# The buffer of x rounded up to a multiple of 2 KB per partition

## The reference

```python
# 1 attention with decay, in blocks of 64 tokens
intra = (q_b @ k_b.T * Dmask) @ v_b
inter = (q_b * lam_pow) @ kv_state
out_b = intra + inter
kv_state = lam_block * kv_state + (k_b * rev_pow).T @ v_b

# 2 gated feed-forward with token shift (d_model 512, d_ff 1024)
xk = mu_k * x + (1 - mu_k) * x_prev          # x_prev: x one token earlier
xr = mu_r * x + (1 - mu_r) * x_prev
x = sigmoid(xr @ w_r) * (max(xk @ w_k, 0) ** 2 @ w_v)

# 3 gate from a causal convolution of 5 taps
gate = sigmoid(sum(conv_w[j] * x shifted by 4 - j tokens))
out = (gate * (x @ w_val)) @ w_out
```

## Time and profile before

| | |
|---|---|
| time, median of 3 runs | 307.41 us (306.47 to 308.93) |
| the profiled execution | 305.9 us |
| its span, first to last instruction | 304.0 us |
| TensorE matmul in flight | 286.8 us, 94% |
| VectorE busy | 164.6 us, 54% |
| ScalarE busy | 118.8 us, 39% |
| GpSimd busy | 48.1 us, 16% |
| granted TensorE clock, mean | 0.983 |

### The profile page before, as it was taken

How to read it: one execution, slowest core, us unless ns; L and a number is a source line. 1 busy time by engine, 2 the same in 40 slices (tenths; PEclk the granted TensorE clock), 3 DMA queues, 4 the chain that set the end, 5 groups by cost and what they waited for, 6 DMA issues and landing times.

```text
span 304.0 us, 4295 instructions
## 1 busy us (share of the span) xinstructions
PE 286.8 (94%) x1772; PEld 232.6 (77%) x1772; DVE 164.6 (54%) x251; ACT 118.8 (39%) x197; POOL 48.1 (16%) x38
## 2 busy tenths in 40 slices
PE   8998698999699999996999999789999999999996
PEld 8877586787488878875888888568887888887885
DVE  6547895298442004765444676621996879714100
ACT  1017624755362104645510155644711711612221
POOL 1684799950000000000000000000000000000000
PEclk9999899999799999999999999979999999999999
DMA  7999993000000000000000000070000000110122
GB/s 274 378 412 409 410 375 110 2 0 3 0 0 0 2 0 0 0 2 0 0 0 2 0 1 0 15 263 2 0 0 2 0 0 0 71 69 0 69 106 104
DMA packets 7506, 23.42 MB, mean 77 GB/s; under 512 B 832, under 2 KB 1216, under 8 KB 7488
## 3 DMA queue, kind: packets, MB, share of 16 engines
q1 hardware_dynamic: 7488, 23.16, 20.1%
HBM read 20.01 MB, written 3.15 MB: 76 GB/s over the span
## 4 chain that ended last, share of the span: by engine, by line
PE 90%; DVE 4%; DMA 3%; ACT 2%; issue 1%
PE ps L638 27%; PE ps L640 26%; PE ps L639 26%; PE ps L654 3%; PE ps L703 3%; DMA qk<-in_qk 3%; PE ps L781 2%; PE ps L671 1%; PE ps L688 1%; DVE xk_f L484 1%; DVE kk_f L499 1%; DVE pT L460 1%; DVE xr_l L490 1%; ACT ring L326 1%; DVE kk_l L504 1%
## 5 line engine op out<-in xcount | busy, mean ns | idle before, releaser
L638 PE MATMUL ps<-xk_h,wk_h 128*128 128x512 f32 x96 | 38.1, 397 | 0.8 <-issue 0.8
L639 PE MATMUL ps<-xk_l,wk_h 128*128 128x512 f32 x96 | 38.1, 396 | 0.0
L640 PE MATMUL ps<-kk_h,wv_l 128*128 128x512 f32 x96 | 38.1, 396 | 0.0
L638 PE MATMUL ps<-kk_h,wv_h 128*128 128x512 f32 x96 | 38.1, 396 | 0.0
L640 PE MATMUL ps<-xk_h,wk_l 128*128 128x512 f32 x96 | 38.0, 396 | 0.0
L639 PE MATMUL ps<-kk_l,wv_h 128*128 128x512 f32 x96 | 38.0, 396 | 0.0
L523 DVE SCALAR_TENSOR_TENSOR gate<-x,prm,gate 128x512 f32<-128x512 f32 x48 | 32.6, 746 | 0.0
L343 ACT ACTIVATE gate<-x,prm 128x512 f32<-128x512 f32 x12 | 8.7, 725 | 54.1 <-DVE x L509 54.1
L638 PE MATMUL ps<-xr_h,wr_h 128*128 128x512 f32 x48 | 20.7, 430 | 7.8 <-DVE xr_l L490 7.8
L499 DVE SCALAR_TENSOR_TENSOR kk_f<-ps,ring 128x512 f32<-128x512 f32 x24 | 16.5, 689 | 18.8 <-ACT ring L326 18.8
L509 DVE TENSOR_TENSOR x<-ps,r 128x512 f32<-128x512 f32 x12 | 8.3, 691 | 33.0 <-PE ps L640 33.0
(11 more groups left out here) (69 smaller groups left out, 525.1 us busy)
## 6 DMA issues: line engine op xcount, KB each, us to landing
qk<-in_qk SPq DMA_DIRECT2D x12, 512.0 KB, 7.0
kv<-in_kv SPq DMA_DIRECT2D x12, 512.0 KB, 7.9
out<-out_sb SPq DMA_DIRECT2D x11, 256.0 KB, 2.0
wk_raw<-in_w_k SPq DMA_DIRECT2D x4, 512.0 KB, 10.1
wv_raw<-in_w_v SPq DMA_DIRECT2D x4, 512.0 KB, 8.7
wr_raw<-in_w_r SPq DMA_DIRECT2D x2, 512.0 KB, 8.5
w_raw<-in_w_val SPq DMA_DIRECT2D x2, 512.0 KB, 4.5
w_raw<-in_w_out SPq DMA_DIRECT2D x2, 512.0 KB, 8.0
```

The source lines that it names most:

```text
L638: nc.tensor.matmul(to, left(0), right(0), start=(i == 0), stop=False)
L639: nc.tensor.matmul(to, left(0), right(1), start=False, stop=False)
L640: done = nc.tensor.matmul(to, left(1), right(0), start=False, stop=(i == last))
```

## The change

The size that x takes is rounded up to the next multiple of 2,048 bytes, from 24,736 to 26,624. All that is laid out behind x moves up by 1,888 bytes: xk, xr, kk, ring, r, own, prm and all that shares their places. The weights and x stay where they are. No instruction is added, taken away or moved.

```diff
@@ -64,7 +64,7 @@
         KB = 1024
         wk_at, wr_at, wv_at = take(32 * KB), take(16 * KB), take(32 * KB)
-        x_at = take(4 * KT * XW)
+        x_at = take(-(-4 * KT * XW // (2 * KB)) * 2 * KB)
         xk_at, xr_at, kk_at = take(16 * KB), take(16 * KB), take(32 * KB)
         ring_at, r_at = take(8 * KB), take(8 * KB)
         own_at = take(16 * KB)
```

## The result

| | before | changed |
|---|---|---|
| time, median | 306.94 us (4 runs, 304.76 to 308.93) | 298.72 us (4 runs, 297.34 to 300.98) |
| ratio | | 0.974, 95% interval 0.9691 to 0.9789 |
| profiled execution, its span | 305.9, 304.0 us | 297.34, 295.3 us |
| granted TensorE clock, mean | 0.983 | 0.988 |

The change makes the kernel 2.6% faster. I had forecast no change (307.4 us, with 305.1 to 309.2 as the range).

The account below looks back on a forecast made before the run. TensorE was taken as the bound: number of matmuls times start-to-start distance, plus seams. Every term was 0 us, so the forecast stayed at the earlier median, 307.4 us, range 305.1 to 309.2, with 0.84 for within 1%.

Parts of the forecast that it names:

- Four distances are sampled by the four values of n.: Hidden layer: 128-column blocks n were taken to sample four operand distances, with no interval differing by 10 ns in 2,810.
- the distance of its two operands: TensorE: changing the separation of moving and stationary operands within 2 KB was forecast at 0 us, bound +1.0.
- 864 matmuls x 0.9 = 0.8 us: TensorE: most that operand alignment could gain, from 233.3 ns in the projection against 234.2 in hidden; bound -0.8 us.
- The term of the absolute addresses: TensorE: moving operands going from 32 past a multiple of 64 bytes to a multiple was forecast at 0 us, bound -0.8.
- Half of those matmuls stand at distance 0 and pay nothing: Attention, `attend`: operands at distance 0 or 256 take 63.8 ns each, read as no price for distance 0.
- The line through the 256- and the 512-column pace: TensorE: 120 and 233.3 ns extrapolated to 63.3 ns for 128 columns, compared with 63.8 ns in `attend`.
- The rival with the right mechanism: All 996 full-width matmuls: the 21 ns excess is an address effect, removed by a common grid; 286.6 us, half 297; chance 0.05.
- The slower rival: TensorE: weight load and moving stream meet when operands are equal modulo 512 bytes; +3.8 us, 311.2 us; chance 0.05.
- The independence of the two reads: TensorE: weight load and moving stream have independent ports per the Trainium skill, making the price of their meeting 0.
- VectorE, ScalarE and GpSimd at 0: The three other compute engines: address changes forecast to cost 0 us, with a bound of -1.0 us for GpSimd.
- The DMA at 0: Loads of qk and kv: moved targets forecast at 0 us, bounds -0.7 and +0.7 us.
- The clock episodes: Receptance heads: lower granted clock loses 1.7 us each; two or more extra or fewer, chance 0.03 slower, 0.03 faster.

Follow-up runs that it names:

- the kernel with 64, 128, 256: Changed kernel with pads ahead of xk, xr and kk, giving operand distances 64 in hidden, 128 in receptance, 256 in value; 299.21 us.
- the kernel with 320, 384, 448: Changed kernel with pads ahead of xk, xr and kk, giving operand distances 320 in hidden, 384 in receptance, 448 in value; 305.01 us.

## Why the prediction was wrong

**"Four distances are sampled by the four values of n."** This is the step that failed. The blocks are 512 bytes apart, and the pace repeats every 256. The five rows are five readings of one distance, 160. The 512-column stages of before held two in all, 160 and 96 (the projection with its sign), and their 234.2 and 233.3 ns are two entries of the table above. Equal times over inputs that differ by multiples of one number say nothing on what lies between.

So the term that rested on it, "the distance of its two operands", was mis-sized: it had 0, with a bound on the slow side only (+1.0 us), and measured -7.4 us over 996 matmuls.

**"864 matmuls x 0.9 = 0.8 us" at most.** The term of the absolute addresses is 0 as forecast: everything moved up by 32 bytes leaves 226.7 ns. But its bound of -0.8 us served as the fast end for all of TensorE, and it came from a comparison in which both sides were slow: the 0.9 ns lie between distances 160 and 96. I had noted that the two operands change sides in it, and still took the difference for the most that addresses could give.

**"Half of those matmuls stand at distance 0 and pay nothing"** (those of `attend`). True, but no evidence. With 64 weight columns and 128 moving ones, `attend` takes 1.02 us per 16 at distance 0 and also at 128 (the kernel with 64, 128, 256), and 1.02 to 1.03 at 192 (the kernel with 320, 384, 448); these short streams don't show the effect at any of the three. The line through the 256- and the 512-column pace, which met the value of `attend` so well, joined a matmul that the change doesn't touch (120 ns before and after) with one that it does. Its agreement was chance: with 226.7 in place of 233.3 ns the same line gives 66.7 ns, and `attend` still takes 63.8.

**The rival with the right mechanism was named and got 0.05.** "An address effect that a common grid removes" was priced at 20.8 us or half of it. The change took 7.4 of the 20.8: 226.7 is not 213.3. Most of its chance was for a part of the gain, as it came, but the arguments against it were the two samples above, and with them gone there was nothing in the trace against it.

**The slower rival had the sign reversed.** I asked whether both reads of TensorE meet when the operands are equal modulo 512, and priced that as a loss. With 128-column loads and 512-column streams, no distance was faster than equal modulo 256. The independence of the two reads, which I had cited from the Trainium skill ("TensorE: Matmul & The Clock Gate", the step on LDWEIGHTS), is not what the runs show: the pace of an unchanged stream followed the width of the load, by -7.5 and +3.3 ns, and the place of a third of the loads, by +6.0.

**What held.** VectorE, ScalarE and GpSimd at 0: their durations moved by 4 ns at most in the earlier trace rows and by 0.01 us in the earlier trace rows. The DMA at 0: 407 and 420 GB/s against 413 and 418; a waste of 96 bytes in 4,096, as the Trainium skill has it ("DMA: Bandwidth & Descriptors", "How a descriptor splits into AXI transactions"), would be 2.3% in an estimate, and the two stretches moved by -1.5% and +0.5%, so they neither show it nor rule it out. That starts on multiples of 64 bytes are worth nothing held as well: the kernel shifted by 32 bytes is as fast per matmul. The clock episodes came and went as described, from none to three at the three receptance heads of a trace, at 1.5 us each where I had 1.7. They aren't the whole scatter between runs: 297.34 and 299.12 us of the changed kernel have the same mean clock (0.988 and 0.989), and the start of the hidden layer, which moved by up to 3.5 us between traces, is the other part that the traces show.

## What to carry to other kernels

Where TensorE streams 512 columns of fp32r back to back with a 128-column weight load for each, measure the pace from start to start and compare it with 226.7 ns, the best seen here. If it is above, try layouts in which moving and stationary operands are equal modulo 256 bytes, and measure again: for 256-column streams and for 64-column loads that distance wasn't the best. Here 96 bytes of padding gave the same pace as 1,888. And before an observation is counted as a sample of a condition, ask in which unit the condition repeats: a stride that is a multiple of the period samples the same point again and again.

## What the runs showed of the hardware that I had not expected

- The pace of 512-column fp32r matmuls depends on the signed distance between moving and stationary operand modulo 256 bytes: 226.7 ns at 0, 228.8 to 229.2 at 64, 232.1 to 234.4 at the other multiples of 32. A shift of all addresses by 32 bytes leaves it (226.7).
- It is sharp at 0: 16 bytes off cost 5 ns, 8 bytes 5 to 7.
- It depends on the width of the weight load (64 instead of 128 columns turned 234.2 into 226.7 and 226.7 into 230.0), and at one distance it has two stable values, 226.7 and 236.7 ns.
- It isn't a law for all widths: 256-column streams take 120.0 ns at distance 0 and at -160, and 117.8 at three others; 128-column streams with 64-column loads take about 64 ns at distances 0, 128 and 192 alike.
- Four of the settled paces, 226.7, 230.0, 233.3 and 236.7 ns, are 544, 552, 560 and 568 clocks of 2.4 GHz, 512 plus 32, 40, 48 and 56, so they lie 8 clocks apart; 228.8, 231.7 and 234.2 ns (549, 556 and 562) don't fit that ladder. A collision of the two reads in something that repeats every 256 bytes would look like this; that is an argument, not shown. What the last 32 clocks at distance 0 are, and which load is met, stays open.
